# An attention and two feed-forward networks on one core: the value products moved one slot sooner, and GpSimd's work redistributed

## The reference

```python
kv_pool = kv.reshape(B, H // 4, 4, W // 4, 4, C).mean(axis=(2, 4))
k = v = kv_pool.reshape(B, -1, C) @ w_sr            # 768 keys of 128
s = (q @ k.transpose(0, 2, 1)) / sqrt(C)
a = exp(s - s.max(-1)); a /= a.sum(-1) + 1e-9
x = (a @ v).reshape(B * S, C)                       # 2 x 12288 tokens
h = x @ moe_w_in;  x = (h * cos(h)) @ moe_w_out                     # 128 -> 2048 -> 128
h = x @ moe2_w_in; y = (h / (1 + exp(-1.702 * h))) @ moe2_w_out
```

## Time and profile before

| | |
|---|---|
| Median of three runs | 2604.05 us |
| The profiled execution's own time | 2606.78 us |
| Its span, first to last instruction | 2605.0 us |
| Mean granted TensorE clock | 0.998 |
| Attention | about 24 to 500 us |
| Joint | about 480 to 545 us |
| Loop over both networks | about 545 us to the end |

### The profile page before, as it was taken

The page is one execution under the profiler, slowest core; times in us unless marked ns, Lnnn a source line. Parts: engine busy times, 40 slices in busy tenths (PEclk is TensorE's granted clock), DMA queues, the critical chain, the costliest instruction groups (busy, mean ns, idle before and its releaser), DMA issues.

```text
span 2605.0 us, 37963 instructions
## 1 busy us (share of the span) xinstructions
PE 2576.3 (99%) x11797; PEld 2130.5 (82%) x11797; DVE 2066.7 (79%) x2264; ACT 1881.6 (72%) x2280; POOL 2174.7 (83%) x1830
## 2 busy tenths in 40 slices
PE   8999999999999999999999999999999999999999
PEld 7887877778888888888888888888888888888887
DVE  8777888887787878787878787777787877787876
ACT  5666777787777777777777777777777777777776
POOL 3878999899888888888888888888888888888883
PEclk9999999999999999999999999999999999999999
DMA  8978888601010101010101010101010101010100
GB/s 244 263 217 239 218 242 233 175 17 25 12 24 12 24 12 24 12 24 12 24 12 24 12 24 12 24 12 24 12 24 12 24 12 24 12 24 12 24 5 13
DMA packets 188844, 156.17 MB, mean 60 GB/s; under 512 B 117296, under 2 KB 142192, under 8 KB 187760
## 3 DMA queue, kind: packets, MB, share of 16 engines
q1 hardware_dynamic: 173904, 126.97, 18.4%
q10 hardware_dynamic: 14880, 28.46, 4.3%
HBM read 54.59 MB, written 25.26 MB: 31 GB/s over the span
## 4 chain that ended last, share of the span: by engine, by line
PE 89%; POOL 8%; DVE 1%; DMA 1%; issue 1%; SPq 1%; ACT 0%; ACTq 0%; POOLq 0%
PE psum L677 28%; PE psum L679 28%; PE psum L678 28%; POOL probs_t_lo L587 5%; PE psum L749 1%; PE psum L751 1%; PE psum L761 1%; POOL g_lo L662 1%; POOL w_lo L616 1%; POOL probs_t_hi L599 1%; PE psum L710 1%; PE psum L779 1%; DVE neg_max L1276 0%; DMA q_blocks<-in_q 0%; SPq L465 0%
## 5 line engine op out<-in xcount | busy, mean ns | idle before, releaser
L662 POOL TENSOR_TENSOR g_lo<-g,g_hi 128x512 fp32r<-128x512 f32 x768 | 1134.9, 1478 | 67.1 <-ACT g_hi L1191 7.1
L1409 DVE TENSOR_TENSOR g_lo<-g,g_hi 128x1024 fp32r<-128x1024 f32 (+1 forms) x396 | 644.7, 1628 | 436.9 <-ACT g L1186 435.1
L1184 ACT ACTIVATE g_hi<-psum 128x1024 fp32r<-128x1024 f32 (+1 forms) x396 | 397.3, 1003 | 559.5 <-PE psum L679 559.5
L659 POOL CAST g_hi<-g 128x512 fp32r<-128x512 f32 x750 | 550.8, 734 | 226.5 <-DVE g L1400 226.5
L677 PE MATMUL psum<-g_hi,w_lo 128*128 128x512 f32 x1536 | 598.1, 389 | 0.8 <-POOL g_lo L662 0.8
L677 PE MATMUL psum<-x_hi,w_lo 128*128 128x512 f32 x1536 | 598.3, 390 | 0.0
L679 PE MATMUL psum<-x_hi,w_hi 128*128 128x512 f32 x1536 | 598.1, 389 | 0.0
L678 PE MATMUL psum<-x_lo,w_hi 128*128 128x512 f32 x1536 | 598.0, 389 | 0.0
L678 PE MATMUL psum<-g_lo,w_hi 128*128 128x512 f32 x1536 | 597.8, 389 | 0.0
L679 PE MATMUL psum<-g_hi,w_hi 128*128 128x512 f32 x1536 | 597.6, 389 | 0.0
L1400 DVE TENSOR_TENSOR g<-psum,g 128x512 f32<-128x512 f32 x768 | 490.0, 677 | 1.9 <-ACT g L1177 1.8
(11 more groups left out here) (87 smaller groups left out, 2464.4 us busy)
## 6 DMA issues: line engine op xcount, KB each, us to landing
gathered<-turned SPq DMA_DIRECT2D x320, 96.0 KB, 3.4
gathered<-turned ACTq DMA_DIRECT2D x192, 96.0 KB, 3.4
gathered<-turned_last SPq DMA_DIRECT2D x160, 96.0 KB, 3.1
x_dram<-x_out SPq DMA_DIRECT2D x48, 256.0 KB, 2.6
x_raw<-x_dram SPq DMA_DIRECT2D x48, 256.0 KB, 2.7
x_inv<-inverse_dram SPq DMA_DIRECT2D x48, 256.0 KB, 3.4
out<-y_blocks SPq DMA_DIRECT2D x190, 64.0 KB, 2.7
q_blocks<-in_q SPq DMA_DIRECT2D x47, 256.0 KB, 3.1
```

The lines of the kernel that those rows point to most:

```text
L659: nc.gpsimd.tensor_copy(g1_hi[at][:, t], g1[at][:, t]).then_inc(g1_hi_ready, 1)
L662: nc.gpsimd.tensor_tensor(g1_lo[at][:, t], g1[at][:, t], g1_hi[at][:, t].bitcast(F32), ALU.subtract).then_inc(g1_lo_ready, 1)
L1184: nc.scalar.activation(g2_hi[ring2(j, p)][:, t], h2[buffer2(j)][:, t], ACT.Silu, scale=GELU)
L1409: nc.vector.tensor_tensor(g2_lo[ring2(j, p)][:, t], g2[ring2(j, p)][:, t], g2_hi[ring2(j, p)][:, t].bitcast(F32), ALU.subtract).then_inc(g ...
```

## The change

It has seven parts.

1. `HI_SLOT`, `LO_SLOT`, `VALUES_SLOT` and `STORE_SLOT` each go down by one: rounding, subtracting, value products and stores of every chunk stand one slot sooner in their engine's stream, while scores, exponentials, transposes and DMA issues keep their slots.
2. For the eight chunks 24, 27, 30, ..., 45 ScalarE rounds the third part as well (`all_by_scalar`), and GpSimd does not.
3. GpSimd's scaling of the first weight goes; ScalarE's rounding applies the factor itself, and VectorE subtracts these four pieces with one `scalar_tensor_tensor` each (scaled raw value less the upper part), in slots 108, 112, 116 and 120.
4. Weight pieces 4 to 15 stay on GpSimd, in the same slots.
5. `round_x1(1, 1, 1)` moves from slot 188 of GpSimd to behind its last subtraction of the attention.
6. The last chunk's lower products (`sum_lower(CHUNKS - 1, ...)`) move from step 4 of the joint to step 5.
7. `store_x1(CHUNKS - 4)` and `sum_values(CHUNKS - 3, PARTS - 1)` now fall inside the slot loop and leave the code behind it.

```diff
-    HI_SLOT, LO_SLOT, VALUES_SLOT, STORE_SLOT = 8, 9, 10, 15
+    HI_SLOT, LO_SLOT, VALUES_SLOT, STORE_SLOT = 7, 8, 9, 14
...
+    def all_by_scalar(c):
+        return c >= CHUNKS - 2 or c >= CB and c % 3 == 0
     def upper_made(engine, c, i):
-        if i == BY_POOL and c < CHUNKS - 2:
-            engine.wait_ge(probs_hi_by_pool, c + 1)
+        whole = sum(all_by_scalar(n) for n in range(c))
+        if i == BY_POOL and not all_by_scalar(c):
+            engine.wait_ge(probs_hi_by_pool, c + 1 - whole)
...
@@ gpsimd
-            def unscale_piece(m):
...
             def split_piece(i):
                 pool.wait_ge(w_hi_ready, i + 1)
+                if i == PIECES_A_WEIGHT:
+                    pool.wait_ge(w_split, PIECES_A_WEIGHT)
...
             for s in range(LO_SLOT, TILES):
                 c, i = divmod(s - LO_SLOT, SUB)
-                if i == 0:
+                if i == 0 and not all_by_scalar(c):
                     round_probabilities(c)
...
-                if (s - UNSCALE_SLOT) % 2 == 0 and 0 <= s - UNSCALE_SLOT < 2 * PIECES_A_WEIGHT:
-                    unscale_piece((s - UNSCALE_SLOT) // 2)
...
-                    if 0 <= i < WEIGHT_PIECES:
+                    if PIECES_A_WEIGHT <= i < WEIGHT_PIECES:
                         split_piece(i)
-                if s == TILES - 4:
-                    round_x1(1, 1, 1)
             for i in range(2):
                 lower_probabilities(CHUNKS - 2, i)
+            round_x1(1, 1, 1)
@@ tensor
-            for i in (PARTS - 1, PARTS):
-                sum_values(CHUNKS - 3, i)
+            sum_values(CHUNKS - 3, PARTS)
...
-                    if r * BODY + p == 4:
+                    if r * BODY + p == 5:
                         sum_lower(CHUNKS - 1, range(KT))
@@ scalar
-                nc.scalar.activation(hi, raw, ACT.Copy).then_inc(w_hi_ready, 1)
+                nc.scalar.activation(hi, raw, ACT.Copy,
+                                     scale=1.0 / GELU if o == 0 else 1.0).then_inc(w_hi_ready, 1)
...
-                if c >= 0 and i < (BY_POOL if c < CHUNKS - 2 else PARTS):
+                if c >= 0 and i < (PARTS if all_by_scalar(c) else BY_POOL):
                     round_probabilities(c, i)
@@ vector
+            def split_piece(i):
+                hi, lo, raw = split_of(i)
+                dve.wait_ge(w_hi_ready, i + 1)
+                nc.vector.scalar_tensor_tensor(lo, raw, 1.0 / GELU, hi.bitcast(F32), ALU.mult,
+                                               ALU.subtract).then_inc(w_split, 1)
...
+                if (s - 2 - SPLIT_SLOT) % SPLIT_GAP == 0:
+                    i = (s - 2 - SPLIT_SLOT) // SPLIT_GAP
+                    if 0 <= i < PIECES_A_WEIGHT:
+                        split_piece(i)
```

More of the change, by code:

```diff
@@ L99, in attention_and_networks @@
     WEIGHT_ORDER = (3, 0, 1, 2)
-    UNSCALE_SLOT, SPLIT_SLOT, SPLIT_GAP = 84, 106, 4
+    SPLIT_SLOT, SPLIT_GAP = 106, 4
     KEY_SLOTS = {SB - 6: 2, SB - 5: 3, SB - 2: 4, SB: 5}
@@ L135, in attention_and_networks @@
     half_pi = put("half_pi", [P, 1], F32)
-    unscale = put("unscale", [P, 1], F32)
     silu_probe = put("silu_probe", [P, 1], F32)
@@ L278, in attention_and_networks @@
     raw_loaded = [sem(f"raw_loaded{n}") for n in range(4)]
-    unscale_made = sem("unscale_made")
-    unscaled = sem("unscaled")
     w_hi_ready = sem("w_hi_ready")
@@ L380, in by_tile @@
         return x.rearrange("p (j a t) -> p a j t", a=GROUPS, j=SUB)
+    def all_by_scalar(c):
+        return c >= CHUNKS - 2 or c >= CB and c % 3 == 0
     def upper_made(engine, c, i):
-        if i == BY_POOL and c < CHUNKS - 2:
-            engine.wait_ge(probs_hi_by_pool, c + 1)
-        else:
-            engine.wait_ge(probs_hi_ready,
-                           c * BY_POOL + i + 1 + (PARTS - BY_POOL if c == CHUNKS - 1 else 0))
+        whole = sum(all_by_scalar(n) for n in range(c))
+        if i == BY_POOL and not all_by_scalar(c):
+            engine.wait_ge(probs_hi_by_pool, c + 1 - whole)
+        else:
+            engine.wait_ge(probs_hi_ready, c * BY_POOL + whole + i + 1)
     def lower_made(engine, c, i):
@@ L564, in _ @@
         def _(pool):
-            nc.gpsimd.memset(unscale[:, :], 1.0 / GELU).then_inc(unscale_made, 1)
             nc.gpsimd.memset(ident[:, :], 0.0).then_inc(ident_made, 1)
@@ L601, in round_probabilities @@
                                       ).then_inc(probs_hi_by_pool, 1)
-            def unscale_piece(m):
-                if m == 0:
-                    pool.wait_ge(unscale_made, 1)
-                    pool.wait_ge(raw_loaded[WEIGHT_ORDER[0]], 16)
-                x = split_of(m)[2]
-                nc.gpsimd.tensor_tensor(x, x, unscale[:, :].to_broadcast([P, WP_COLS]),
-                                        ALU.mult).then_inc(unscaled, 1)
             def split_piece(i):
@@ L1084, in round_weights @@
                     act.wait_ge(values_summed, CB)
-                    act.wait_ge(unscaled, PIECES_A_WEIGHT)
-                elif i % PIECES_A_WEIGHT == 0:
+                if i % PIECES_A_WEIGHT == 0:
                     act.wait_ge(raw_loaded[WEIGHT_ORDER[o]], 16)
                 hi, _, raw = split_of(i)
-                nc.scalar.activation(hi, raw, ACT.Copy).then_inc(w_hi_ready, 1)
+                nc.scalar.activation(hi, raw, ACT.Copy,
+                                     scale=1.0 / GELU if o == 0 else 1.0).then_inc(w_hi_ready, 1)
             def copy_tile(n):
@@ L1161, in _ @@
             regroup(CHUNKS - 1, 0)
-            store_x1(CHUNKS - 4)
             regroup(CHUNKS - 1, 1)
```

## The result

The changed kernel takes 2610.49 us in the median (2606.01 to 2613.55, 16 runs); the kernel before, run beside it, 2605.33 (2602.25 to 2611.32, 16 runs). The ratio is 1.0016, interval 1.0009 to 1.0022: 0.16% slower, inside the 0.2% that I called no change, but outside noise, and 5.2 us from the kernel before where I had forecast -1.5. It lies 0.5 us above the top of my range. A later session gave 1.0007 (0.9998 to 1.0016) for the same kernel, so its true cost is some 2 to 5 us, with intervals that together reach from 0 to 6; by that session's median, 2608.08 us, it would lie inside my range. The profiled execution took 2612.23 us (span 2610.5), 5.45 more than the one before.

What follows compares the result with a forecast made beforehand. TensorE was taken as busy 99% of the span, with GpSimd the bound from 325 to 390 us. Terms -9.3 + 3.5 + 4.0 + 2.4 + 0.9 - 3.0 = -1.5 us gave 2602.5 us, range 2594 to 2610.

Steps and rivals of the forecast that it cites:

- GpSimd relieved: Attention: less GpSimd work per chunk ends 15 waits of lower products, 0.64 us each, less 0.3 left over: -9.3 us.
- Four pieces on VectorE: Attention: four weight pieces of about 2 us each on VectorE delay what is queued behind them: +3.5 us (0 to 5.5).
- Gathers at 31 and 35: Chunks 31 and 35: gathers behind weight loads land too late for the sooner slot, 2 us each: +4.0 us.
- Chunk 18: Two weights load at once, ScalarE already waits for the gather, so the slot is paid in full: +2.4 us (1.2 to 4).
- Early chunks: Chunks 0 to 2: sooner rounding on ScalarE holds up the queries' rounding; 0.4 and 0.5 us: +0.9 us (0 to 2.5).
- The joint: Five TensorE waits for GpSimd and VectorE go, 5.9 us, but VectorE is late next: -3.0 us (0 to -6).
- A late gather makes the next one late: Rival, after the weight loads: waiting roundings delay the next chunk's issues, two more chunks late each: 2610.4 us, chance 0.12.
- Cover holds: Rival, attention: gathers at 31 and 35 cause no wait and VectorE's pieces fit: 2595.1 us, chance 0.27.
- GpSimd stays the bound: Rival, attention: relief doesn't reach TensorE after chunk 28, -6.0 in place of -9.3: 2605.8 us, chance 0.08.

Runs made afterwards that it cites:

- the change again: The changed kernel itself, unaltered, run and profiled a second time: 1.0007 (0.9998 to 1.0016) of the kernel before.
- the best version: The change with parts 1 and 7 undone, GpSimd's weight pieces behind the third subtraction, weights loaded behind gathers of chunks 18, 20, 31, 35: 0.9949, 2593.36 us.
- Pieces last, alone: The kernel before with only GpSimd's 16 weight pieces moved behind a chunk's third subtraction: 0.9983 (0.9974 to 0.9992).
- slots back: The change with part 1, and part 7 that follows from it, undone: 0.9983 (0.9974 to 0.9992) of the kernel before.
- pieces back on GpSimd: The change with part 3 undone, GpSimd scaling and subtracting pieces 0 to 3 of the first weight again: 0.9997 (0.9988 to 1.0006).
- rounding last: The change with ScalarE's rounding of probabilities last in its slot, behind the exponentials, queries' rounding and DMA issues: 1.0053 (1.0039 to 1.0067).
- slot sooner only: The kernel before with parts 1 and 7 of the change alone: 0.9995 (0.9986 to 1.0004).
- all bulk loads behind a gather: The change with weight and row loads issued behind the regrouping: 1.0000; also with old slots and GpSimd's pieces behind the third subtraction: 0.9978.
- weights' loads spread: The change with weights loaded behind gathers of chunks 18, 20, 31, 35: 0.9979; with old slots and pieces behind the third subtraction: 0.9949.

## Why the prediction was wrong

The direction was wrong: -1.5 us forecast, +5.2 measured (+2.7 in the later session). By the table, the profiled execution lost 3.7 us more than forecast from 340 to 455 (the gathers at 31 and 35), 2.9 more in the early chunks and 2.3 more in the joint, and 2.0 less at chunk 18 and at the pieces. In the change again the first two came out within 1 us of the forecast; the joint was 2.2 off once more. So two steps failed. One is the price of a late gather, where I left out the fall of the clock that follows; how much it costs differs from one execution to the next. The other, in both executions, is the joint, which I let gain 3.0 us while the slot took its cover away. Term by term, from the profiled execution:

**GpSimd relieved, -9.3.** About right in size. Every wait of a lower product from 300 to 445 is gone and chunks are 8.90 us apart; the best version, in which little else disturbs, gains 8.0 us from 245 to 455. But I credited most of it to less work, and the piece's place only with a lead. Pieces last, alone, gains 3.9 us from 285 to 455 with the work unchanged, and slots back with the same relief still waits eight times. So about half is the place: the piece stood ahead of the subtraction that TensorE waits for. The other half comes from ScalarE's third roundings, without which the best version gains only 3.6 there by its trace (its median is 2.1 us apart). VectorE's four pieces add nothing to it: with them on GpSimd, the third roundings kept and the pieces last, the gain is 8.9.

**Four pieces on VectorE, +3.5.** Right in size: each made its chunk 9.76 us long, 0.86 over 8.90, 3.4 in all. Wrong in two details: a piece took 1.44 us, not 2, because it began 1.5 us into a subtraction of 2.4, and TensorE waited 0.67 us for the copy of inverses, not for the exponentials. With the slots put back the four begin beside GpSimd's short rounding or its idle time, and cost 0.5 to 1.0 us of waits in all; so they cost what they do because of the slot.

**Gathers at 31 and 35, +4.0.** The waits were 1.96 and 2.09 us, as worked out. What failed is the words "with the restart 0.26": each wait was followed by a half-clock stretch of 3.41 us, 1.7 us of work each, 3.4 in all. With it the four chunks around the two waits took 7.9 us more than 8.90 each. I had left the clock as it was everywhere, though the kernel before shows a stretch right behind its own wait at chunk 18. In this execution that is the largest single miss. In the change again the waits were 0.71 and 1.65, there was one stretch, and the same four chunks took 5.0 us more.

**Chunk 18, +2.4.** TensorE waited 4.00 for 2.61 us; between 110 and 285 the trace loses 0.9. Both kernels pay one stretch there.

**Early chunks, +0.9 (0 to 2.5).** Measured +3.8. I took ScalarE's and VectorE's order as the price and costed gathers 1 and 2 at 0.5 us. The gather of chunk 2 landed 15.2 us after its last transpose, where it took 13.2 before. A 512 KB row load of SyncE stands ahead of each of the first gathers, as a weight does at 18, 31 and 35, and I didn't look at those; whether they are the cause stays open, as said above. The delay varies: in the eight profiles with the slot sooner and the row loads in place it is 0.5 to 5.5 us at 110, median 3.2; in the seven with the old slots 0.1 to 5.2, median 0.6. So the slot costs some 2.6 us here, an estimate from the two medians.

**The joint, -3.0.** Measured -0.7. Of the six other profiles with the slot sooner and both of the joint's moves four lie between -0.8 and 0.0, and two lost 0.7 (pieces back on GpSimd) and 2.7 (rounding last), while the seven with the joint's moves and the old slots gained 1.7 to 4.1. So the slot takes back what the moves give. One half-clock stretch of the two that the joint had before is gone, too, which is 1.7 us that I hadn't counted; without it the joint would have lost 1.0. These are the rows of VectorE's g, of ScalarE's last rounding and of TensorE:

```profile
508.36 1.21 DVE L1380 SCALAR_TENSOR_TENSOR g<-turns,psum 128x1024 f32<-128x1024 int32 x1
...
511.56 2.94 ACT L1031 ACTIVATE probs_t_hi<-gathered 128x1024 fp32r<-128x1024 f32 x3
...
512.75 0.66 PE L738 MATMUL psum<-probs_t_hi,v_lo 128*128 128x512 f32 x1 [2.60 <-ACT probs_t_hi L1031]
```

The last chunk's rounding stands behind the first steps of `g`, which the slot doesn't make sooner. TensorE, which has one slot less of value products left to fill that time (part 7), waits 2.60 us; with the slots put back it waits 0.64 at the same place. I had moved the products in the sum and not what they covered. That the missing products are the reason was read from the two traces and not tried by itself.

**The rivals.** "A late gather makes the next one late" named almost the measured number, 2610.4, but didn't happen: behind the waits at 18, 31 and 35 no rounding of the next two chunks waits for its gather. "Cover holds" asked for pieces of 0.7 us; I saw that only where GpSimd was idle. "GpSimd stays the bound" is what happens with the slots put back and the piece still ahead of the third subtraction.

So the slot sooner is what makes the change slow. How much it costs depends on what stands beside it. Four pairs of kernels differ in it alone, with GpSimd's pieces behind the third subtraction in both (in the first pair the scaling of the first weight keeps its slots, and so moves against the subtractions):

| pair | old slots | slot sooner | difference, us |
|---|---|---|---|
| the kernel before with pieces last | 0.9983 | 0.9995 | 3.1 |
| the change, all bulk loads behind a gather | 0.9978 | 1.0000 | 5.7 |
| the change, weights' loads spread | 0.9949 | 0.9979 | 7.8 |
| the change itself, loads as they were | 0.9965 | 1.0016 (1.0007 again) | 13.3 (10.9) |

Each difference is uncertain by some 3 to 4 us. The first pair, the smallest, has neither VectorE's pieces nor the joint's moves; it says too why slot sooner only wasn't slow: it gained from the piece's place what the slot cost. The third pair's traces, 9.4 us apart at 545, put the price at 3.0 early, 2.4 from 300 to 340 (the pieces), 2.5 in the joint, and 1.5 in the rest.

## What to carry to other kernels

Before work is taken off an engine that bounds a stretch, see which of its instructions is waited for, and move the others behind it: that alone gave about half of the relief here. A stage moved sooner must be paid where its input is latest, so list every bulk transfer issued ahead of such an input on its queue, in all parts of the kernel, and count what the moved work used to cover at the end. Look also at what a moved instruction comes to run beside: the same VectorE piece took from 0.67 to 2.67 us. A wait of TensorE of about 2 us is to be priced with the half-clock stretch that may follow it, and small differences are read from medians of many runs, with the profile for the mechanism alone.

## What the runs showed of the hardware

**A VectorE instruction with two inputs in SBUF beside GpSimd.** The piece took 0.67 us when GpSimd was idle. These are one of the change and one of rounding last, each with the subtraction that was under way and, for the second, the next one:

```profile
302.43 2.42 POOL L586 TENSOR_TENSOR probs_t_lo<-gathered,probs_t_hi 128x1024 fp32r<-128x1024 f32 x1 [0.44 <-ACT probs_t_hi L1031]
303.98 1.42 DVE L1306 SCALAR_TENSOR_TENSOR w_lo<-w_raw,w_hi 128x512 fp32r<-128x512 f32 x1
...
306.56 2.40 POOL L586 TENSOR_TENSOR probs_t_lo<-gathered,probs_t_hi 128x1024 fp32r<-128x1024 f32 x1 [0.80 <-ACT probs_t_hi L1031]
306.83 2.67 DVE L1306 SCALAR_TENSOR_TENSOR w_lo<-w_raw,w_hi 128x512 fp32r<-128x512 f32 x1
308.92 2.81 POOL L586 TENSOR_TENSOR probs_t_lo<-gathered,probs_t_hi 128x1024 fp32r<-128x1024 f32 x1
```

The first piece begins 1.55 us into the subtraction, the second 0.27 us, and both end 0.55 us behind the subtraction's end; so do all eight pieces of these two profiles, to 0.01 us. The next subtraction takes 2.80 to 2.85 us for 2.4. So the piece stands almost still until GpSimd's instruction is through, and then holds up the next one for a part of its own time. The Trainium skill, "SBUF — State Buffer", "Who interferes with whom", says that such a pair contends for a port pair that is locked exclusively. These rows agree, and the 2.67 us is near the most that the prediction worked out from that rule.

**The clock after short waits.** In the change and the change again half-clock stretches came as 3.41 or 6.83 us, at TensorE's waits of 1.65, 1.96, 2.09, 2.60 us and more; none came at a wait of 0.71. The wait of 2.60 us in the joint had one and that at chunk 2 of the profiled change had none. Over the 18 profiles, between 30 us and the end of the networks, a stretch began during the wait or within 2 us behind it for all 11 waits of 3.3 us and more, for 17 of the 24 from 1.9 to 2.9, for 5 of the 15 from 1.5 to 1.9, and for 3 of the 49 from 1.0 to 1.5. So a wait of about 2 us makes a stretch likely in this kernel, not certain; what decides it wasn't tried. In the best version, without a wait over 1.5 us from 40 us to the end of the joint, there is none.

**Order of issue on one queue.** With SyncE's weights behind a gather in place of ahead, the gather landed 4.4 to 7.6 us sooner, and what stood behind the weights, the query rows, became late. The Trainium skill, "DMA: Bandwidth & Descriptors", "Queues, rings and completion order", says that each DMA engine consumes the descriptors of one issuer's ring in order. The trace agrees: the delay moved with the order and went nearly away when the two loads were issued two chunks apart: TensorE's wait for query rows was 3.6 to 4.5 us in the four kernels with both weights behind chunk 18, and 1.1 us or none in the three with the second weight behind chunk 20.
